# The TensorE program of a convolution and two MLPs: a repeated stretch written out, or put in a hardware loop

## What is computed

```python
def _attn_ref(x, weight):              # x 2 x 4096 x 192, weight 8 x 7
    w = softmax(weight, axis=-1)       # seven taps for each of 8 groups of 24 channels
    ...                                # causal convolution along the sequence, zeros ahead
    out = np.einsum('hk,bskhg->bshg', w, x_unf)

def _moe_ref(x, w_in, w_out):          # 8192 tokens, 192 -> 2048 -> 192
    h = x @ w_in
    g = np.maximum(0.01 * h, h)
    return g @ w_out

def _moe2_ref(x, w_in, w_out):         # the same sizes, another activation
    h = x @ w_in
    g = np.where(h >= 1, h, np.where(h <= -1, 0.0, (h + 1) ** 2 / 4))
    return g @ w_out

return _moe2_ref(_moe_ref(_attn_ref(x, weight)))
```

## Time and profile before

| | before |
|---|---|
| median of 3 runs | 1163.86 us (1163.84 to 1165.13) |
| the profiled execution | 1163.84 us, of which 1162.1 us lie between its first and last instruction (the span) |
| PE matmuls | 1152.9 us busy (99%), x9764 |
| PE weight loads | 929.9 us (80%), x9764 |
| DVE | 896.3 us (77%) |
| ACT | 798.6 us (69%) |
| granted PE clock | 0.999 of full speed |
| instruction packets, queue q8 | 77, 1.26 MB |
| instruction packets, queue q14 | 72, 0.59 MB |

### The profile page before, as it was taken

The page is one execution under the profiler, slowest core; times in us unless marked ns, Lnnn a source line. Parts: engine busy times, 40 slices in busy tenths (PEclk is TensorE's granted clock), DMA queues, the critical chain, the costliest instruction groups (busy, mean ns, idle before and its releaser), DMA issues.

```text
span 1162.1 us, 25804 instructions
## 1 busy us (share of the span) xinstructions
PE 1152.9 (99%) x9764; PEld 929.9 (80%) x9764; DVE 896.3 (77%) x1509; ACT 798.6 (69%) x1473; POOL 50.6 (4%) x76
## 2 busy tenths in 40 slices
PE   9999999999999999999999999999999999999998
PEld 7878888888888888888888888888888888888886
DVE  6788777888777887788877787777787877878665
ACT  6768667586675857758577685766758567685685
POOL 5560000000000000000000000000000000000000
PEclk9999999999999999999999999999999999999999
DMA  5420010101001010010100101001010100100001
GB/s 138 111 62 2 11 19 1 29 2 19 11 1 30 2 28 2 1 30 1 28 2 8 24 1 29 1 15 17 1 29 1 26 6 1 29 1 15 1 1 28
DMA packets 114469, 22.19 MB, mean 19 GB/s; under 512 B 106128, under 2 KB 114320, under 8 KB 114320
## 3 DMA queue, kind: packets, MB, share of 16 engines
q1 hardware_dynamic: 114000, 20.07, 9.4%
q10 hardware_dynamic: 320, 0.26, 0.1%
HBM read 14.02 MB, written 6.29 MB: 17 GB/s over the span
## 4 chain that ended last, share of the span: by engine, by line
PE 94%; DVE 2%; ACT 2%; SPq 1%; issue 0%; POOL 0%; DMA 0%; POOLq 0%; ACTq 0%
PE hidden L385 15%; PE hidden L377 10%; PE acc_edge L441 10%; PE acc_main L447 10%; PE hidden L381 10%; PE hidden L379 10%; PE acc_main L449 10%; PE acc_main L451 10%; PE acc_edge L438 10%; DVE g L843 1%; ACT g_hi L644 0%; SPq L261 0%; ACT pre L625 0%; SPq L268 0%; DVE acc_main L781 0%
## 5 line engine op out<-in xcount | busy, mean ns | idle before, releaser
L644 ACT CAST g_hi<-g 128x512 fp32r<-128x512 f32 x512 | 300.0, 618 | 287.0 <-PE acc_main L479 246.2
L854 DVE TENSOR_TENSOR g_lo<-g,g_hi 128x512 fp32r<-128x512 f32 x512 | 335.9, 690 | 122.2 <-ACT g_hi L644 117.4
L385 PE MATMUL hidden<-op_edge,w_edge 64*128 64x512 f32 x768 | 260.7, 393 | 0.0
L848 DVE SCALAR_TENSOR_TENSOR g<-hidden,pre 128x512 f32<-128x512 f32 x256 | 176.6, 690 | 105.7 <-ACT pre L632 102.4
L377 PE MATMUL hidden<-op_hi,w_main 64*128 64x512 f32 x512 | 201.4, 393 | 1.2 <-DVE g L843 0.9
L401 PE MATMUL hidden<-op_hi,w_main 64*128 64x512 f32 x512 | 201.5, 394 | 0.0
L397 PE MATMUL hidden<-op_hi,w_main 64*128 64x512 f32 x512 | 201.5, 394 | 0.0
L441 PE MATMUL acc_edge<-g_lo,w_out 64*128 64x512 f32 x508 | 200.0, 394 | 1.1 <-DVE g_lo L854 0.8
L381 PE MATMUL hidden<-op_hi,w_main 64*128 64x512 f32 x512 | 201.0, 393 | 0.0
L399 PE MATMUL hidden<-op_lo,w_main 64*128 64x512 f32 x512 | 201.0, 393 | 0.0
L404 PE MATMUL hidden<-op_edge,w_edge 64*128 64x512 f32 x512 | 201.0, 393 | 0.0
(11 more groups left out here) (111 smaller groups left out, 2787.9 us busy)
## 6 DMA issues: line engine op xcount, KB each, us to landing
x_in<-in_x_dram SPq DMA_DIRECT2D x68, 64.0 KB, 2.2
out_dram<-y_main SPq DMA_DIRECT2D x64, 64.0 KB, 1.9
stage<-in_moe_w_out_dram SPq DMA_DIRECT2D x16, 192.0 KB, 2.7
x_in_edge<-in_x_dram SPq DMA_DIRECT2D x68, 32.0 KB, 1.9
out_dram<-y_edge SPq DMA_DIRECT2D x32, 64.0 KB, 1.8
stage<-in_moe_w_in_dram SPq DMA_DIRECT2D x15, 128.0 KB, 2.3
stage<-in_moe_w_in_dram SPq DMA_DIRECT2D x30, 64.0 KB, 2.4
stage<-in_moe_w_in_dram ACTq DMA_DIRECT2D x1, 128.0 KB, 3.2
```

The lines of the kernel that those rows point to most:

```text
L385: done = nc.tensor.matmul(h[:], w_edge[l][top, i - 3, cols], op_edge[l][b][top, :], start=False, stop=False)
L644: nc.scalar.copy(g_hi[c % SLOTS][:], g[c % SLOTS][:]).then_inc(g_hi_ready, 1)
L854: nc.vector.tensor_tensor(g_lo[c % SLOTS][:], g[c % SLOTS][:], g_hi[c % SLOTS][:].bitcast(F32), ALU.subtract).then_inc(g_lo_ready, 1)
```

## The change

PE runs its jobs through `all_jobs` too. The two first and two last jobs stay written out; the seven passes become a loop on PE whose body is the four jobs of `loop_jobs`, with the loop's counter in a PE register and the values of the waits worked out from it. The matmuls, their order and what they wait for are the same. The other engines' programs are untouched.

```diff
@@ -589,13 +589,7 @@
             keep_warm(WARM_ON[1])
-            for job in first_jobs:
-                run(job)
-            for j in range(PASSES):
-                for job in loop_jobs(j):
-                    run(job)
-            for job in last_jobs:
-                run(job)
+            all_jobs(pe, run)
             for i in range(10):
                 bottom_second(last_jobs[-1], CHUNKS - 6, i)
```

## The result

The changed kernel takes 1183.85 us (median of 4 runs, 1181.87 to 1184.83), the kernel before 1164.49 us (median of 4). The ratio is 1.017, interval 1.0155 to 1.0183: slower, by 19.4 us. The forecast was 1178.8 in a range of 1170 to 1192. The profiled execution took 1185.6 us, 1.75 above the median.

What follows compares the result with a forecast made beforehand. PE was taken as the bound, without slack. Each of six taken branches idles it 3.3 + 0.2 - 1.0 = 2.5 us, 15 us in all, so 1163.84 + 15 = 1178.8 us; range 1170 to 1192.

Steps and rivals of the forecast that it cites:

- What bounds the kernel: Between first jobs and end: PE busy 99% of the span, no gap in a 141.87 us pass, so stalls are paid in full.
- The taken branch: At PE's loop end: the long body's start is fetched from memory again, 3.3 us each, bounds 2.6 and 3.7.
- What hides a part: At PE's branch: matmuls already handed over keep PE going, a cover of 1.0 us, between 0.7 and 1.6.
- The restart: Behind PE's branch: one register operation of 0.07 us and the first load within 0.1, together 0.2 us.
- at clock 1.00: Expected sign in the profile: 2.5 us gaps in PE's matmuls ahead of L377, six places, at full clock.
- the bubbles: Rival: register operations at L447's wait don't fit, each pair of chunks gets a bubble; 1201 us, or 1433 at worst; chance 0.16.
- Register arithmetic: On PE's sequencer: at most 1.2 us of wait-value operations per pair of chunks, beside the matmuls, costed at nothing.
- The tightest place: PE's wait at L447, released at 225.0, needed at 225.27: 0.5 us for one register operation and three matmuls, enough.
- A hidden fetch, not slower: Rival at PE's branch: body start kept or queue deeper, so the fetch costs nothing, 1163.8 us; chance 0.06.
- Two fetches a branch: Rival at PE's branch: body starts near a block's end, the next block is needed at once; 35 us, 1199; chance 0.04.

Runs made afterwards that it cites:

- 4 runs: Not a follow-up run: a count, the four timed runs behind the median of the changed kernel, 1183.85 us; the kernel before has 1164.49 us (median of 4).
- The announced branch: Changed kernel with PE's loop announcing its branch target (`hint_back_edge=True`), register arithmetic kept: 1165.07 us.
- The filler runs: Changed kernel with 11, in a second run 4, extra matmuls at the end of each pass, ahead of PE's branch: 1186.82 us and 1180.75 us.
- The loops of PE alone: Separate kernel, none of the reference: PE loops of five iterations without waits, bodies of 40 to 1216 matmuls; taken branch 0.21 us up to 840, 3.3 to 3.7 from 960.
- the 960-matmul loop: One loop in a separate kernel with PE alone, no waits, five iterations, body of 960 matmuls; its four taken branches each have a second gap, 1.1 to 1.5 us.
- the changed kernel's two profiles: The changed kernel as first measured, 1183.85 us, and the same kernel run once more beside the follow-up runs, 1184.39 us.
- the kernels with two and one taken branches: Changed kernel with one pass written out, then three iterations of two passes: 1172.13 us; with five passes written out, then two iterations: 1168.04 us.

## Why the prediction was right, and where it wasn't

*What bounds the kernel* held: PE has no slack, so each stall is paid in full, and nothing was gained.

*The taken branch* held in kind. The announced branch shows it: 3.59 us go to 0.44, and the whole cost goes with them. Its size was estimated from ACT's 2.7 and the longer packet as 3.3, with a bound of 3.7; it is 3.59 in the median, and the six taken ones go from 3.39 to 3.74. (The 0.9 in that bound doesn't come out of its row: three times q14's 0.37 is 1.1.) I had expected q8 to stay at about 77 packets; it has 15 more (92), so each taken branch brings in two or three of them again.

*What hides a part* was sized too low. I took 1.0 out of 0.7 to 1.6. The branch starts at 226.0, and without it the next load would have come at 227.25: 1.25 us. The point holds that the register operation behind the wait of L447 keeps the sequencer from running far ahead: the last L479 ahead of it ends at 225.26 + 0.39 = 225.65 (row of its matmul), and the register operation on L396 comes at 225.7. Where nothing waits, the cover is 2.1 us. What I had too slow is the step from there: nine matmuls are handed over between 225.7 and the loop's own register operation at 225.9, so in 0.2 to 0.3 us, where I had 0.4 to 0.9. *The restart* is 229.87 - 229.6 = 0.27 instead of 0.2.

The two errors cancel: 3.61 + 0.27 - 1.25 = 2.6 where the forecast had 3.3 + 0.2 - 1.0 = 2.5. That the gap came out so close is luck in part.

*The step that was missing* is the clock. The forecast expected the gaps "at clock 1.00", with no term for it. Behind some of the gaps PE runs at 1.2 GHz for 3.4 us, which costs 1.55 us each time, four times in the profiled execution: 6.2 us, and with it 1178.8 becomes 1185.0, against 1185.6 for that execution and a median of 1183.85. PE's busy time, forecast at about 1152.9, is 1161.6 for the same reason (6.2 of the 8.7). Without this term the forecast's own mechanism ended at 1183. The measured time is inside the range only because I had widened it to 1192 for the bubbles, which don't exist: that is luck. The filler runs show that it is the idle stretch: shortened from 2.56 to 1.37 or 0.35 us it leaves the clock alone, in both runs. The loops of PE alone, without fillers, agree: 52 idle stretches of 1.1 to 1.75 us, no drop. Why a gap of 2.5 us is followed by a drop at one branch and not at the next is open.

*Register arithmetic* costed at nothing held, by the announced loop: 1165.07, the pass 141.87. The tightest place, L447, makes no bubble, and the hand-over rate of at most 0.05 us a matmul is at the fast end of my 0.04 to 0.117; the nine matmuls above went faster still.

*The rivals.* A hidden fetch, not slower: refuted. Its condition was a cover of 3.1 us; it is 1.25 here, and 2.1 where nothing waits. (With 11 slower fillers queued it is 3.6, and there the fetch is hidden.) The Trainium skill, page "Advanced Engine Details and Errata", section "Engine Queue Depths", has 64 for PE, from which I had estimated 3.7 us; the measured 2.1 us at 0.117 a matmul are 18 matmuls or 36 instructions. Bubbles: refuted, as said. Two fetches a branch: not seen in this kernel, each pass has one gap; but they exist, as the second gaps of the 960-matmul loop show. The Trainium skill, page "Runtime: NRT & Kernel Launch", section "Instruction fetch mechanics", gives PE 2048 instructions; the edge measured here, which decides, lies between 1680 and 1720. For this body of 2432 and more both say the same.

## What to carry to other kernels

On the engine that bounds a kernel, a hardware loop with a long body costs a fetch at each taken branch, less only what the queue holds; on an engine with slack the same loop is free. Look at the register operation and branch rows of the engines that already loop, since they give the price before one moves the bound engine into a loop. If the loop is wanted, for a smaller program, announce its target at the top of the body, or keep the body short enough to stay; and count with the clock wherever PE gets a new idle stretch of over 2 us (here 2.2 to 2.7 us were followed by a drop in ten places of fifteen).

## What the runs showed that I had not expected

- The clock drops above: idle stretches of 2.2 to 2.7 us of the weight loads are followed by 3.4 us at half clock in some places (four of six and three of six in the changed kernel's two profiles, both of the two and the one in the kernels with two and one taken branches), those of 1.1 to 1.75 us in none. The length alone doesn't decide it: one of 2.23 us was followed by a drop and one of 2.54 wasn't.
- With the loop, PEld is busy 96% of the span instead of 80%, at the same 141.87 us a pass (the announced loop: 1135.3 us of PEld against 929.9). Before, the loads of the top and the bottom rows start together every 0.233 us. In the changed kernel they start one by one every 0.117 us, and not only from the first branch on but from the loop's first loads at 85.49, behind a stall of 1.0 us. What sets this off wasn't tried. Twenty per cent more busy time of the weight loads meant nothing for the pace.
- What ends a wait by the profile was wrong at the place that mattered: 13.8 us are put down to DVE's `g`; 12.7 of them (six gaps of 2.1) were the branch.
